# Start-up of a fused recurrent attention and two-layer MLP kernel: paced first loads, spare matmuls between the first levels, an earlier diagonal

## The reference

```python
for t in range(S):
    cur = einsum('bhd,bhe->bhde', u * k[t], v[t])
    y[t] = einsum('bhd,bhde->bhe', r[t], state + cur)
    state = w[t][..., None] * state + einsum('bhd,bhe->bhde', k[t], v[t])
x = y as [3072, 384]
h = x @ w_in;  g = h if h >= 1, 0 if h <= -1, else (h + 1)**2 / 4;  x = g @ w_out
h = x @ w_in2; g = h if h > 0, else exp(h) - 1;                     out = g @ w_out2
```

## Time and profile before

| | us |
|---|---|
| median of three runs | 1022.08 (1021.9 to 1022.91) |
| the profiled execution | 1023.31 |
| its span, first to last instruction | 1021.5 |
| PE busy | 989.6 |
| DVE, ACT, POOL busy | 554.2, 517.4, 46.7 |

### The profile page before, as it was taken

How to read it: one execution, slowest core, us unless ns; L and a number is a source line. 1 busy time by engine, 2 the same in 40 slices (tenths; PEclk the granted TensorE clock), 3 DMA queues, 4 the chain that set the end, 5 groups by cost and what they waited for, 6 DMA issues and landing times.

```text
span 1021.5 us, 25102 instructions
## 1 busy us (share of the span) xinstructions
PE 989.6 (97%) x11080; PEld 812.3 (80%) x11080; DVE 554.2 (54%) x824; ACT 517.4 (51%) x926; POOL 46.7 (5%) x44
## 2 busy tenths in 40 slices
PE   4799899999999999999999999999999999999998
PEld 4788888777777777787778888888888888888886
DVE  5687877667666766776643454433433333333332
ACT  3465356454635354545456775554445444444543
POOL 5830000000000000000000000000000000000000
PEclk9899999999999999999999999999999999999999
DMA  9622032032002203020206000000000001000000
GB/s 327 200 79 96 24 121 110 3 141 78 33 28 115 80 33 115 28 80 33 95 1 216 1 31 31 32 21 11 32 31 1 31 32 31 31 1 1 31 1 31
DMA packets 24699, 61.71 MB, mean 60 GB/s; under 512 B 2448, under 2 KB 6928, under 8 KB 24592
## 3 DMA queue, kind: packets, MB, share of 16 engines
q1 hardware_dynamic: 24592, 60.12, 16.7%
HBM read 50.68 MB, written 9.44 MB: 59 GB/s over the span
## 4 chain that ended last, share of the span: by engine, by line
PE 90%; DVE 4%; POOL 2%; issue 1%; ACT 1%; DMA 1%; SPq 0%; ACTq 0%; DVEq 0%; POOLq 0%
PE down_banks L576 39%; PE up_bank L576 29%; PE g_banks L576 17%; PE y_bank L576 3%; DVE att L1025 1%; POOL win_lo L515 1%; PE y_bank L628 1%; DMA scratch<-w_in_dram 1%; PE y_bank L710 1%; POOL r_nat L525 0%; DVE r_nat L1054 0%; DVE att L1007 0%; DVE att L1037 0%; DVE ynat L1075 0%; DVE ynat L1078 0%
## 5 line engine op out<-in xcount | busy, mean ns | idle before, releaser
L576 PE MATMUL down_banks<-g_hi,wout_lo 128*128 128x512 f32 (+1 forms) x624 | 246.1, 394 | 0.0
L576 PE MATMUL down_banks<-g_hi,wout_hi 128*128 128x512 f32 (+1 forms) x624 | 235.9, 378 | 0.0
L576 PE MATMUL down_banks<-g_lo,wout_hi 128*128 128x512 f32 (+1 forms) x624 | 235.5, 377 | 0.0
L821 ACT CAST g_hi<-scratch 128x512 fp32r<-128x512 f32 (+1 forms) x192 | 116.0, 604 | 188.8 <-PE down_banks L576 118.9
L1096 DVE TENSOR_TENSOR g_lo<-scratch,g_hi 128x512 fp32r<-128x512 f32 (+1 forms) x192 | 128.4, 669 | 108.6 <-ACT g_hi L821 107.0
L576 PE MATMUL up_bank<-x_hi,win_lo 128*128 128x512 f32 (+1 forms) x480 | 182.6, 380 | 3.0 <-DVE g_lo L1096 1.8
L576 PE MATMUL up_bank<-x_lo,win_hi 128*128 128x512 f32 (+1 forms) x480 | 179.5, 374 | 0.0
L576 PE MATMUL up_bank<-x_hi,win_hi 128*128 128x512 f32 (+1 forms) x480 | 179.4, 374 | 0.0
L576 PEld LDWEIGHTS down_banks<-g_hi,wout_lo 128*128 128x128 f32 x624 | 117.8, 189 | 23.6
L576 PEld LDWEIGHTS down_banks<-g_hi,wout_hi 128*128 128x128 f32 x624 | 117.9, 189 | 23.3
L576 PEld LDWEIGHTS g_banks<-att 64*64 64x64 f32 (+1 forms) x5184 | 105.5, 136 | 36.2 <-issue 20.5
(11 more groups left out here) (98 smaller groups left out, 1075.6 us busy)
## 6 DMA issues: line engine op xcount, KB each, us to landing
att<-rT_dram SPq DMA_DIRECT2D x12, 512.0 KB, 4.0
att<-kT_dram SPq DMA_DIRECT2D x12, 512.0 KB, 5.6
att<-wT_dram SPq DMA_DIRECT2D x12, 512.0 KB, 6.5
r_nat<-rN_dram SPq DMA_DIRECT2D x12, 384.0 KB, 6.7
k_nat<-kN_dram SPq DMA_DIRECT2D x12, 384.0 KB, 7.7
att<-vN_dram SPq DMA_DIRECT2D x12, 384.0 KB, 6.9
x_dram<-r_nat SPq DMA_DIRECT2D x18, 256.0 KB, 2.3
ynat<-x_dram SPq DMA_DIRECT2D x6, 768.0 KB, 4.3
```

Of the source, the lines that this page charges most:

```text
L576: return nc.tensor.matmul(out, lhsT, rhs, start=start, stop=stop, **kw)
L821: return nc.scalar.copy(out, in_)
```

## The change

SP issues its first loads a few at a time, with waits for earlier ones to land between them, and with the tiles of group 1 ahead of pieces 13 to 20. The pieces that were staged in `y` and `scores_` get buffers of their own (`extra`, `outer`), so some waits of `STAGED_BEHIND` go. POOL does `times_keys(0)` and `times_bonus(0)` behind piece 2, the memset behind piece 5, and `diagonal_output(0)` behind piece 6, ahead of `times_keys(1)` and pieces 7 to 18, and no longer waits there for piece 8. PE multiplies zeros (`keep_busy`) before level 0, behind each level of group 0 and around `turn_x`. DVE does mask(l-1) behind update(l), in the place of mask(l). ACT does a small copy first, so that its table is loaded then. The size of the scratch area for descriptors of dynamic DMAs is set to 2048.

```diff
-STAGED_BEHIND = {**{i: 5 for i in range(9, 14)}, 18: 2, 19: 8, 20: 8, 22: 16, 23: 17, 24: 18, 25: 22, 26: 23, 27: 21}
+STAGED_BEHIND = {18: 2, 22: 16, 23: 17, 24: 18, 25: 22, 26: 23, 27: 21}
+IDLE_AFTER_LEVEL = (5, 5, 5, 5, 5, 5, 3)
...
+        outer = sb("outer", [P, 5, DM])
+        extra = sb("extra", [P, 3, TOK])
+        idle_work = x_lo[1][:, 0, :]
...
+            def landed(i):
+                sp.wait_ge(piece_in[STAGE[i]], 16)
             load_channels(0)
             load(masks_d, masks[:, :, :].rearrange("p l t -> p (l t)"), masks_in)
-            load_pieces(range(0, 3))
-            load_natural(0, 0)
+            load_pieces(range(0, 1))
+            sp.wait_ge(rk_in[0], 32)
+            load_pieces(range(1, 3))
+            sp.wait_ge(w_in[0], 16)
+            load_natural_r(0, 0)
+            landed(0)
+            load_natural_k(0, 0)
+            landed(1)
             load(uN, u_nat[:, :], bonus_in)
-            load_pieces(range(3, 6))
+            landed(2)
+            load_pieces(range(3, 4))
+            load_pieces(range(4, 5))
+            sp.wait_ge(nat_in[0], 32)
+            load_pieces(range(5, 6))
             load(vN[0, 0], v_[0], v_in[0])
-            load_natural(0, 1)
-            load_pieces(range(6, 9))
+            landed(3)
+            load_natural_r(0, 1)
+            landed(4)
+            load_natural_k(0, 1)
+            landed(5)
+            load_pieces(range(6, 7))
+            sp.wait_ge(v_in[0], 16)
+            load_pieces(range(7, 8))
+            load_pieces(range(8, 9))
             load(ident_d, ident[:, :], ident_in)
-            load_pieces(range(14, 19))
-            load_pieces(range(9, 14))
-            load_channels(1)
-            load_pieces(range(19, 21))
+            sp.wait_ge(nat_in[1], 32)
+            load_pieces(range(9, 11))
+            landed(6)
+            load_pieces(range(11, 12))
+            landed(7)
+            load_pieces(range(12, 13))
+            landed(8)
+            load(rT[0, 1], r_[1], rk_in[1])
+            landed(9)
+            landed(10)
+            load(kT[0, 1], k_[1], rk_in[1])
+            landed(11)
+            landed(12)
+            load(wT[0, 1], w_[1], w_in[1])
+            sp.wait_ge(rk_in[1], 32)
+            load_pieces(range(13, 17))
+            sp.wait_ge(w_in[1], 16)
+            load_pieces(range(17, 21))
...
-                pool.wait_ge(w1_lo_ready, 9 if g == 0 else 21)
+                if g == 1:
+                    pool.wait_ge(w1_lo_ready, 21)
...
-            for i in range(6):
+            for i in range(3):
                 lo_of_weights(i)
             times_keys(0)
             times_bonus(0)
+            for i in range(3, 6):
+                lo_of_weights(i)
+            pool.wait_ge(w1_lo_ready, 6)
+            nc.gpsimd.memset(near[1], 0.0).then_inc(scores_zeroed[1], 1)
+            lo_of_weights(6)
+            diagonal_output(0)
             times_keys(1)
-            for i in range(6, 9):
-                lo_of_weights(i)
-            diagonal_output(0)
-            for i in range(9, 14):
-                lo_of_weights(i)
-            pool.wait_ge(w1_lo_ready, 14)
-            nc.gpsimd.memset(near[1], 0.0).then_inc(scores_zeroed[1], 1)
-            for i in range(14, 19):
+            for i in range(7, 19):
                 lo_of_weights(i)
...
+            def keep_busy(n):
+                for _ in range(n):
+                    mm(up_bank[1][:, :], idle_work[:, 0:P], idle_work)
+            pe.wait_ge(idle_work_ready, 1)
+            keep_busy(8)
             for l in range(NL):
                 pair_products(0, 0, l)
+                keep_busy(IDLE_AFTER_LEVEL[l])
             for b in range(2):
                 attend(0, b)
             turn_k(0, 0)
-            for b in range(2):
-                turn_x(0, b)
+            keep_busy(2)
+            turn_x(0, 0)
+            keep_busy(2)
+            turn_x(0, 1)
+            keep_busy(4)
...
             act.wait_ge(consts_ready, 1)
+            copy(table_loaded[:, :], consts[:, 0:1])
...
+            nc.vector.memset(idle_work.bitcast(F32), 0.0).then_inc(idle_work_ready, 1)
             nc.vector.memset(near[0], 0.0).then_inc(scores_zeroed[0], 1)
...
                 update(0, 0, l)
-                mask(0, 0, l)
+                if l:
+                    mask(0, 0, l - 1)
                 next_decays(0, 0, l)
...
-    nc = bacc.Bacc("TRN2", target_bir_lowering=False, num_devices=1)
+    nc = bacc.Bacc("TRN2", target_bir_lowering=False, num_devices=1, dynamic_dma_scratch_size=2048)
```

More of the change, by code:

```diff
@@ L76 @@
             W1_OUT[11:13] + W1_IN[3][2:3] + W1_OUT[13:16]
-STAGE = ["g0", "g1", "q", "scores0", "scores1", "scores2", "y0", "y1", "y2",
-         "scores_0", "scores_1", "scores_2", "scores_3", "scores_4", "v0", "v1", "state0", "state1",
+STAGE = ["g0", "g1", "q", "scores0", "scores1", "scores2", "extra0", "extra1", "extra2",
+         "outer0", "outer1", "outer2", "outer3", "outer4", "v0", "v1", "state0", "state1",
          "q", "y_0", "y_1", "keys", "state0", "state1", "q", "state0", "state1", "keys"]
-STAGED_BEHIND = {**{i: 5 for i in range(9, 14)}, 18: 2, 19: 8, 20: 8, 22: 16, 23: 17, 24: 18, 25: 22, 26: 23, 27: 21}
+STAGED_BEHIND = {18: 2, 22: 16, 23: 17, 24: 18, 25: 22, 26: 23, 27: 21}
 IDLE_PIECES = 9, 17
+IDLE_AFTER_LEVEL = (5, 5, 5, 5, 5, 5, 3)
 PIECES_OF_SLOT = {0: (17, 18), **{f: (18 + f,) for f in range(1, 10)}}
@@ L138, in build @@
                    **{f"scores{i}": a_[1][:, i * TOK:(i + 1) * TOK] for i in range(3)},
-                   **{f"scores_{i}": a_[1][:, i * DM:(i + 1) * DM] for i in range(5)},
-                   **{f"y{i}": ynat_flat[:, i * TOK:(i + 1) * TOK] for i in range(3)},
+                   **{f"outer{i}": outer[:, i, :] for i in range(5)},
+                   **{f"extra{i}": extra[:, i, :] for i in range(3)},
                    **{f"y_{i}": ynat_flat[:, (2 + i) * DM:(3 + i) * DM] for i in range(2)},
@@ L148, in build @@
         consts = sb("consts", [P, 3])
+        table_loaded = sb("table_loaded", [P, 1])
+        idle_work = x_lo[1][:, 0, :]
         up_bank = [bank(f"up_bank{i}") for i in range(2)]
@@ L193, in build @@
         consts_ready = sem("consts_ready")
+        idle_work_ready = sem("idle_work_ready")
         scores_zeroed = [sem(f"scores_zeroed{g}") for g in range(2)]
```

## The result

The changed kernel takes 1026.29 us (median of 5 runs, 1025.26 to 1027.55) against 1022.09 us before (1021.9 to 1023.11): ratio 1.0038, interval 1.0023 to 1.0052. It is slower, by 4.2 us in the medians. Its profiled execution took 1025.52 us with a span of 1023.7, 2.2 us over the profiled one of before, so that is what its trace has to account for; the other 2 us of the medians no trace shows. The prediction was 1016.5, range 1013 to 1021, with 0.80 on faster.

The account below looks back on a forecast made before the run. Bound: the chain of alternating PE and DVE work before the dense matmuls, up to 52.88 us. Gains 2.0 + 4.2 - 0.3 = 5.9, less 0.3 for a short clock fall: 1022.08 - 5.6 = 1016.5 us, range 1013 to 1021.

Parts of the forecast that it names:

- Part 4: SP's held-back loads: no gain, cost 0 to 2 us, taken as 0.3, at 330 to 380 GB/s.
- half-of-it rival: Pieces come 2 us late or the clock falls once between levels: gain 2.5 to 3.5 us, about 1019; chance 0.20.
- Part 5: From T (first feed-forward matmul) to group 1's level 3: full clock makes it 13.5 us, not 17.7; gain 4.2.
- Part 2: Group 0's levels: later masks join the chain, costing 4.4 us, which cancels the clock's 4.4 us gain.
- two charges: Added to group 0's levels: 0.4 us for level 0 at the low clock, 0.5 for DVE meeting POOL at the port.
- Part 3: POOL's earlier diagonal: output starts at 29.1 instead of 31.12, 2.0 us earlier, putting the first feed-forward matmul at 33.2.
- Part 1: Spare matmuls around group 0's levels: free at full clock, holding it saves 0.79 us in each of levels 0 to 4.
- slower case: Masks cost their 4.4 us and the clock is not released during the levels: 1025 us; chance 0.08.
- What would show it wrong: Signs: level products at 1.93 us, ACT's high part waiting for a piece, updates of 2.4 us, T above 35.

Follow-up runs that it names:

- c1: b2 with the change's paced load list, nothing else different: 1025.39 us, ratio 1.0022 to the kernel before.
- c2: c1 with pieces 13 to 16 issued ahead of group 1's tiles, every other pace kept: 1020.23 us, ratio 0.9974 to the kernel before.
- b2: b1 plus seven spare matmuls in slot 17, where PE waits for an output: 1017.86 us, ratio 0.9948 to the kernel before.
- a3: The changed kernel with both the loads and the mask order undone: 1019.43 us, ratio 0.9970 to the kernel before.
- b1: a3 plus six spare matmuls in each of slots 1 and 2 of group 1: 1018.49 us, ratio 0.9952 to the kernel before.
- c3: b2 with the mask behind the next level's update, as in the change: 1020.47 us, ratio 0.9978 to the kernel before.
- a1: The changed kernel with SP's loads back in the earlier, unpaced order: 1025.11 us, ratio 1.0013 to the kernel before.

## Why the prediction was wrong

In the change's trace level 3 of group 1 stands at 54.94, where the forecast had 33.2 + 13.5 = 46.7. Of these 8.2 us, 1.7 are there when the output starts (30.80 instead of 29.1), 2.8 come between it and T (6.85 us instead of 4.1), and 3.8 behind T (17.3 us instead of 13.5).

**Part 4, the loads: the step that failed most.** I took 330 to 380 GB/s from the bytes that SP's waits leave in flight, and group 1's tiles by 26. Measured: 248 to 302 GB/s from 10 us on, group 1's keys landed at 30.66, piece 13 at 34. I had added up bytes, but the list is a chain of round trips: each `landed` waits for a load of 2.7 to 6.1 us from issue to landing (kT 4.94), and the next issue comes only then. I had priced the whole pacing at 0.3 us with 2 us as the bound, and the place of pieces 13 to 16, behind the wait for group 1's keys, not at all; c1 puts the pacing at 7.6 us, and c2 puts 4.9 of them down to that place. That the pacing would bring the first keys no sooner was right: they are used at 5.78, in before at 5.87 and in the unpaced b2 at 5.81. The half-of-it rival named the event ("the pieces come 2 us late") but not its size.

**Part 5, the clock behind T.** 4.2 us were to come from a full clock from T to level 3. Measured: 17.3 us for that way, against 17.7 before. Two things failed here. In the change the first low stretch, from 38.0, follows PE's wait ahead of T, so it is the late piece again. But a3 has no such wait and needs 17.1 us too: holding the clock ahead of T did not hold it behind, because PE still idles there (1.66 us at 36.9) and the clock is low from 40.7. I had that in the earlier trace rows and even wrote that PE idle preceded the fall at 48.8, and still took the new clock as 1.00, with 0.3 us off for a short fall. b1 shows that the term was there to be had: 14.1 us.

**Part 2 and its two charges.** The mask on the chain was right in kind and size: the products came 3.84, 3.22 and 3.25 us apart at levels 2 to 5 (predicted 3.77, 3.20, 3.20); in time c3 measured 3.1 us for it, less than the 4.4 counted. The charges were too small. For level 0 and the port I took 0.9 us; level 0 to 1 took 4.29 (2.57 predicted) and 1 to 2 4.37 (3.77), 2.3 us over together. Most of it, 1.7 us, is level 0 at the low clock with its five spare matmuls, for which I had taken 0.4. The port cost the chain little: the update of level 1 took 1.45 us instead of 1.23, and the extra 1.0 us of the decays was hidden, since DVE idled 0.78 us behind them. A fall of the clock during the levels (a1 and c3 at 25 to 30 us) I had only as the rivals' premise.

**Part 3.** The diagonal is done at 29.95 and no longer sets the output, as forecast; the output starts at 30.80, 0.3 us earlier than before instead of 2.0, because the levels took longer, and ACT's pieces then made that worthless.

**Part 1** was right: 3.78 us for the first eight, done before the keys landed; five in 1.42 to 1.45 us at the full clock (1.17 counted), still inside the gaps; levels from the third on at 1.13 us. That a3, without the two damaging parts, has T at 32.86, next to the forecast 33.2, and a best run of 1016.06, next to 1016.5, is chance: the forecast had the late masks in it, the median of a3 is 1019.43, and level 3 came 17.1 us behind T.

**The rivals.** The slower case had 0.08, for a clock that stays low in the levels. That is not what happened in the profiled execution; it was late loads, and the low clock behind T. "What would show it wrong" named it: ACT's high part of x waiting for a piece, and T above 35. The chance for slower should have been carried by that transfer, on which a whole list of new waits depended.

## What to carry to other kernels

When loads are held back until earlier ones land, cost the list as a chain of round trips, issue by issue, and look for the consumer that needs the last of them: here four pieces behind one wait were worth 5 us. Spare work ahead of T did not keep the clock up in the gaps behind it (a3), spare work put into these gaps did (b1, b2), and once the clock was low it did not bring it back in time (c1); so follow PE's gaps to where dense work begins. And two parts of a change may each be worth nothing until the other is in. Compare such kernels over many runs with the granted clock of each beside its time: one trace can lie over 4 us from the median (a3: 1023.82 against 1019.43).

## What the runs showed of the hardware that was not expected

The record of the granted clock says 1.00 at the start, whatever the clock: the first products took 1.93 us under that 1.00 in the change and in before, and 1.15 under the same 1.00 in b2's execution, so that level 0 is at either clock with the same code. With the same levels and the same spare matmuls the clock held in the profiled execution of the change and fell, from about 24.2 on, in those of c3 and a1. A DVE instruction with two inputs in SBUF took 1.73 us instead of 0.73, or 2.42 instead of 1.23, beside a POOL instruction that reads SBUF (for the 2.42, POOL's ran from 46.51 to 48.33 and DVE's ended 1.1 us after it); the Trainium skill (SBUF — State Buffer, SBUF: two separate sides) calls this an exclusive lock, and these durations agree.
